# Chunk sums of log decays and angles: one fp32 product each, or two one-pass products of split parts

## The reference

```python
mag = np.sqrt(a_re * a_re + a_im * a_im)
scale = np.minimum(mag, 0.999) / (mag + 1e-06)
a_re_n, a_im_n = (a_re * scale, a_im * scale)
for t in range(S):                      # S = 768; batch 4, heads 8, head size D = 48
    new_re = ar * S_re - ai * S_im
    new_im = ar * S_im + ai * S_re
    S_re, S_im = (new_re + kv, new_im)  # kv = outer(k_t, v_t)
    y[:, :, t] = q_t @ S_re
```

## Time and profile before

| | us |
|---|---|
| median of 3 runs | 878.79 (877.34 to 878.93) |
| the profiled execution | 878.05 |
| its span, first to last instruction | 876.3 |
| PE busy | 830.9 (95% of the span) |
| DVE busy | 357.0 |
| ACT busy | 347.1 |
| POOL busy | 160.6 |
| mean granted clock of TensorE | 0.985 |

### The profile page before, as it was taken

The page is one execution under the profiler, slowest core; times in us unless marked ns, Lnnn a source line. Parts: engine busy times, 40 slices in busy tenths (PEclk is TensorE's granted clock), DMA queues, the critical chain, the costliest instruction groups (busy, mean ns, idle before and its releaser), DMA issues.

```text
span 876.3 us, 13204 instructions
## 1 busy us (share of the span) xinstructions
PE 830.9 (95%) x5194; PEld 744.6 (85%) x5194; DVE 357.0 (41%) x668; ACT 347.1 (40%) x606; POOL 160.6 (18%) x193
## 2 busy tenths in 40 slices
PE   1499999999999799999999999999999999999997
PEld 0277887798899589999998989998999889988997
DVE  1598878868765422223413122132122122122112
ACT  6889988888652131111112222222222222222221
POOL 2101122712503305555300001001001001001001
PEclk9699999999999899999999999999999999999999
DMA  9999778666523496899720001000000000000001
GB/s 171 160 205 244 105 99 123 113 94 83 136 94 117 140 202 167 266 233 252 224 73 1 1 0 37 1 1 37 1 1 36 1 1 37 1 1 37 0 1 37
DMA packets 174165, 77.31 MB, mean 88 GB/s; under 512 B 151592, under 2 KB 167304, under 8 KB 174096
## 3 DMA queue, kind: packets, MB, share of 16 engines
q1 hardware_dynamic: 169168, 60.54, 34.4%
q0 software_dynamic: 4928, 15.84, 6.4%
HBM read 60.80 MB, written 15.59 MB: 87 GB/s over the span
## 4 chain that ended last, share of the span: by engine, by line
PE 91%; DVE 3%; issue 2%; ACT 2%; DMA 1%; POOL 0%; SPq 0%; DVEq 0%; ACTq 0%; POOLq 0%
PE f_pU L1698 23%; PE f_pO L1704 22%; PE e_pH L1434 9%; PE e_pY L1448 8%; PE sc L515 5%; PE kvp L529 3%; PE tq L497 2%; PE tk L502 2%; PE yp L540 2%; PE yp L542 2%; PE cs L472 2%; PE cs L110 2%; PE cs L485 1%; PE cs L486 1%; PE cs L92 1%
## 5 line engine op out<-in xcount | busy, mean ns | idle before, releaser
L1698 PE MATMUL f_pU<-f_xT,wi 128*128 128x512 f32 x864 | 215.1, 395 | 0.8 <-DVE f_xT L1639 0.8
L1704 PE MATMUL f_pO<-wo,gT 128*128 128x384 f32 x1152 | 213.8, 336 | 0.0
L1704 PEld LDWEIGHTS f_pO<-wo,gT 128*128 128x128 f32 x1152 | 202.6, 188 | 7.5
L1698 PEld LDWEIGHTS f_pU<-f_xT,wi 128*128 128x128 f32 x864 | 161.3, 188 | 32.5 <-DVE f_xT L1639 1.2
L1655 DVE TENSOR_TENSOR gT<-g,gT 128x512 fp32r<-128x512 f32 x96 | 66.5, 692 | 286.5 <-ACT gT L1682 286.5
L1677 ACT ACTIVATE g<-f_pU 128x512 f32<-128x512 f32 x96 | 57.5, 599 | 298.3 <-PE f_pU L1698 298.3
L1645 POOL DMA_INDIRECT out<-o,row_of x24 | 24.1, 1004 | 420.8 <-DVE o L1666 414.4
L1434 PE MATMUL e_pH<-e_xT,ring 128*128 128x224 f32 x384 | 75.8, 358 | 0.1
L1434 PEld LDWEIGHTS e_pH<-e_xT,ring 128*128 128x128 f32 x384 | 74.0, 194 | 0.7 <-issue 0.3
L1448 PE MATMUL e_pY<-hT,ring 128*128 128x224 f32 x384 | 74.1, 353 | 0.0
L1448 PEld LDWEIGHTS e_pY<-hT,ring 128*128 128x128 f32 x384 | 72.1, 190 | 0.0
(11 more groups left out here) (196 smaller groups left out, 1007.6 us busy)
## 6 DMA issues: line engine op xcount, KB each, us to landing
ring<-in_moe_w SPq DMA_DIRECT2D x16, 1536.0 KB, 9.6
ring<-in_a_re SPq DMA_DIRECT2D x8, 576.0 KB, 8.8
ring<-in_a_im SPq DMA_DIRECT2D x8, 576.0 KB, 8.9
ring<-in_q SPq DMA_DIRECT2D x8, 576.0 KB, 8.1
ring<-in_k SPq DMA_DIRECT2D x8, 576.0 KB, 8.2
vraw<-in_v SPq DMA_DIRECT2D x8, 576.0 KB, 5.4
xs<-zero SPq DMA_DIRECT2D x9, 343.9 KB, 7.1
part<-in_moe_w_in POOLq DMA_DIRECT2D x12, 256.0 KB, 6.3
```

What stands on the lines that cost most here:

```text
L1698: mm = pe.matmul(pU[f % 2][:, :], wi[:, pw, c, f * 128:(f + 1) * 128], xT[b % 2][:, px, c, :], start=(k == 1), stop=(k == NK * len(TERMS)))
L1704: mm = pe.matmul(pO[t][:, 0:DM], gT[f % GB][:, pg, t * 128:(t + 1) * 128], wo[:, pw, f, :], start=(f == 0 and k == 0), stop=(f == NF - 1 a ...
```

## The change

The log decays (from group 2 on) and the angles (from group 1 on) are no longer multiplied in fp32. POOL splits each tile into a rounded fp32r part and the rest (LH, LL and AH, AL); PE multiplies both by a triangle `tri_r` in fp32r and adds them up in PSUM. The product with `pone` stays in fp32. The angles are first multiplied by 1/2pi on POOL, after `prefix` has read them. LH and LL lie where FD and FI lie. The tile ZZ is gone: its readers and writers use FD, the two exponentials that are run for their sums write to LM and GI. With that come new waits: `log_growth(g)` waits for qf_done of g (FD of the last group read by DVE) and for `fend_out` of g groups; `size_sum` waits for the split of the last group; the second part of the split waits for kf_done; `sum_l` and `sum_phi` wait for POOL. SP's program is not touched.

```diff
--- before.py
+++ after.py
@@ -234,7 +234,7 @@
 
 def attention(nc, sem, q, k, v, a_re, a_im, X, ident, cst, routing, w_skip, w_gate, xs, ends_dram, stat, fend_all, flag,
               ring, load_unit):
-    F32 = mybir.dt.float32
+    F32, F32R = mybir.dt.float32, mybir.dt.float32r
     ALU = mybir.AluOpType
     ACT = mybir.ActivationFunctionType
     PI = float(np.pi)
@@ -266,13 +266,19 @@
     DP = HALF + D
     PAIRS = HG // 2
     SWAPPED = LAST - NC
+    SPLIT_L, SPLIT_A = 2, 1
+    TURN = 0.5 / PI
+
+    def angles(g):
+
+        return (NC - 1) * g + 3 * max(g - SPLIT_A, 0)
 
     cols = [t.rearrange("b h (c p) d -> p (b h c) d", p=C) for t in (a_re, a_im, q, k, v)]
 
     ctx = ExitStack()
     with ctx:
-        def sb(name, shape, dt=F32):
-            return ctx.enter_context(nc.sbuf_tensor(name, shape, dt))
+        def sb(name, shape, dt=F32, stack=ctx):
+            return stack.enter_context(nc.sbuf_tensor(name, shape, dt))
 
         def pb(name, shape):
             return ctx.enter_context(nc.psum_tensor(name, shape, F32))
@@ -284,6 +290,9 @@
 
         NN = sb("NN", [128, W])
         FR = sb("FR", [128, W])
+        with ExitStack() as parts_ctx:
+            LH = sb("LH", [128, W], F32R, parts_ctx)
+            LL = sb("LL", [128, W], F32R, parts_ctx)
         FD = sb("FD", [128, W])
         FI = sb("FI", [128, W])
         zero = sb("zero", [SUB, X.shape[2]])
@@ -297,7 +306,10 @@
         GI = sb("GI", [128, W])
         WW = sb("WW", [128, W])
         LM = sb("LM", [128, W])
-        ZZ = sb("ZZ", [128, W])
+        ZZ = FD
+        AH = sb("AH", [128, W], F32R)
+        AL = sb("AL", [128, W], F32R)
+        tri_r = sb("tri_r", [128, C], F32R)
         AT = sb("AT", [128, HG, NC, D])
         PRE = sb("PRE", [128, HG, NC, D])
         xT = [sb(f"r_xT{i}", [128, DM])[:, :] for i in range(2)]
@@ -326,7 +338,7 @@
         kvp = pb("kvp", [128, 512])
 
         names = """re_in0 re_in1 im_in0 im_in1 qk_in0 qk_in1 v_in0 v_in1 fend_out fend_in0 fend_in1 const_ok blank_done
-            lr_done g_done w_done w2_done lw_done lm_done z_done l_done at_done pre_done size_done spread_done
+            lr_done split_l g_done w_done w2_done lw_done lm_done z_done l_done at_done pre_done size_done spread_done
             wg_blank wg_in route_const xT_done xT_out logit_done step chosen hot_done run_done rank_done slot_done sent
             limits_done count_done table_done good_step good_done sum_good flag_done
             sum_l sum_phi f_done rnd_done fr_done abs_done cos_done sin_done qf_done kf_done front_done back_done
@@ -427,6 +439,29 @@
                                pattern=[[-1, 128]], channel_multiplier=1).then_inc(s["const_ok"], 1)
             pool.wait_ge(s["const_ok"], 3)
             routing.constants(pool, s)
+            pool.tensor_copy(tri_r[:, :], tri[:, :]).then_inc(s["const_ok"], 1)
+
+            def split_l(g):
+
+                if g < SPLIT_L:
+                    return
+                pool.wait_ge(s["l_done"], g + 1)
+                pool.tensor_copy(LH[:, :], LM[:, :]).then_inc(s["split_l"], 1)
+                pool.wait_ge(s["split_l"], 2 * (g - SPLIT_L) + 1)
+                pool.wait_ge(s["kf_done"], g)
+                pool.tensor_tensor(LL[:, :], LM[:, :], LH[:, :], ALU.subtract).then_inc(s["split_l"], 1)
+
+            def split_a(g):
+
+                if g < SPLIT_A:
+                    return
+                at = AT[:, :, :, :].rearrange("p h c d -> p (h c d)")
+                pool.wait_ge(s["pre_done"], angles(g + 1) - 3)
+                pool.tensor_scalar(at, at, TURN, None, ALU.mult).then_inc(s["pre_done"], 1)
+                pool.wait_ge(s["pre_done"], angles(g + 1) - 2)
+                pool.tensor_copy(AH[:, :], at).then_inc(s["pre_done"], 1)
+                pool.wait_ge(s["pre_done"], angles(g + 1) - 1)
+                pool.tensor_tensor(AL[:, :], at, AH[:, :], ALU.subtract).then_inc(s["pre_done"], 1)
 
             def prefix(g):
                 pool.wait_ge(s["at_done"], g + 1)
@@ -434,13 +469,15 @@
                     pool.wait_ge(s["sum_phi"], NPC * g)
                 pool.tensor_copy(PRE[:, :, 1, :], AT[:, :, 0, :]).then_inc(s["pre_done"], 1)
                 for c in range(2, NC):
-                    pool.wait_ge(s["pre_done"], (NC - 1) * g + c - 1)
+                    pool.wait_ge(s["pre_done"], angles(g) + c - 1)
                     pool.tensor_tensor(PRE[:, :, c, :], PRE[:, :, c - 1, :], AT[:, :, c - 1, :], ALU.add)\
                         .then_inc(s["pre_done"], 1)
 
             for p in periods():
                 if here(p + 2):
+                    split_l(p + 2)
                     prefix(p + 2)
+                    split_a(p + 2)
                 if p == 3:
                     pool.wait_ge(s["blank_done"], 16 * routing.BLANKS)
                 if p in (3, 5, 7):
@@ -460,7 +497,10 @@
             def sum_l(g, j):
                 if not here(g):
                     return
-                pe.wait_ge(s["l_done"], g + 1)
+                if g < SPLIT_L:
+                    pe.wait_ge(s["l_done"], g + 1)
+                else:
+                    pe.wait_ge(s["split_l"], 2 * (g - SPLIT_L + 1))
                 if j == 0:
                     if g > 0:
                         pe.wait_ge(s["fr_done"], NPC * (g - 1) + 2)
@@ -469,20 +509,31 @@
                         pe.wait_ge(s["fr_done"], NPC * g)
                 else:
                     pe.wait_ge(s["f_done"], NPC * g + 1)
-                pe.matmul(cs[j % 2][:, 0:PW], tri[:, :], piece(LM, j), start=True, stop=True).then_inc(s["sum_l"], 1)
+                bank = cs[j % 2][:, 0:PW]
+                if g < SPLIT_L:
+                    pe.matmul(bank, tri[:, :], piece(LM, j), start=True, stop=True).then_inc(s["sum_l"], 1)
+                    return
+                pe.wait_ge(s["const_ok"], 4)
+                pe.matmul(bank, tri_r[:, :], piece(LH, j), start=True, stop=False)
+                pe.matmul(bank, tri_r[:, :], piece(LL, j), start=False, stop=True).then_inc(s["sum_l"], 1)
 
             def sum_phi(g, j):
                 if not here(g):
                     return
                 at, pre = (t[:, :, :, :].rearrange("p h c d -> p (h c d)") for t in (AT, PRE))
                 pe.wait_ge(s["at_done"], g + 1)
-                pe.wait_ge(s["pre_done"], (NC - 1) * (g + 1))
+                pe.wait_ge(s["pre_done"], angles(g + 1))
                 if j < 2:
                     pe.wait_ge(s["f_done"], NPC * g + 2 + j)
                 else:
                     pe.wait_ge(s["fr_done"], NPC * g + 1)
                 bank = cs[(NPC + j) % 2][:, 0:PW]
-                pe.matmul(bank, ptri[:, :], at[:, j * PW:(j + 1) * PW], start=True, stop=False)
+                if g < SPLIT_A:
+                    pe.matmul(bank, ptri[:, :], at[:, j * PW:(j + 1) * PW], start=True, stop=False)
+                else:
+                    pe.wait_ge(s["const_ok"], 4)
+                    pe.matmul(bank, tri_r[:, :], piece(AH, j), start=True, stop=False)
+                    pe.matmul(bank, tri_r[:, :], piece(AL, j), start=False, stop=False)
                 pe.matmul(bank, pone[:, :], pre[:, j * PW:(j + 1) * PW], start=False, stop=True)\
                     .then_inc(s["sum_phi"], 1)
 
@@ -664,19 +715,23 @@
 
             def size_sum(g):
                 act.wait_ge(s["lr_done"], g + 1)
-                if g > 0:
-                    act.wait_ge(s["l_done"], g)
-                act.activation(ZZ[:, :], LR[:, :], ACT.Exp, accum_out=stat[:, G + g:G + g + 1]).then_inc(s["size_done"], 1)
+                if 0 < g <= SPLIT_L:
+                    act.wait_ge(s["sum_l"], NPC * g)
+                elif g > 0:
+                    act.wait_ge(s["split_l"], 2 * (g - SPLIT_L))
+                act.activation(LM[:, :], LR[:, :], ACT.Exp, accum_out=stat[:, G + g:G + g + 1]).then_inc(s["size_done"], 1)
 
             def spread_sum(g):
                 act.wait_ge(s["w2_done"], g + 1)
-                act.wait_ge(s["l_done"], g + 1)
-                act.activation(ZZ[:, :], GI[:, :], ACT.Exp, scale=SPREAD, accum_out=stat[:, 2 * G + g:2 * G + g + 1])\
+                act.activation(GI[:, :], GI[:, :], ACT.Exp, scale=SPREAD, accum_out=stat[:, 2 * G + g:2 * G + g + 1])\
                     .then_inc(s["spread_done"], 1)
 
             def log_growth(g):
                 act.wait_ge(s["w2_done"], g + 1)
                 act.wait_ge(s["size_done"], g + 1)
+                if g > 0:
+                    act.wait_ge(s["qf_done"], g)
+                    act.wait_ge(s["fend_out"], 16 * g)
                 act.activation(ZZ[:, :], GI[:, :], ACT.Ln, bias=ONE).then_inc(s["lw_done"], 1)
 
             def loss(g):
@@ -687,7 +742,7 @@
             def angle(g):
                 if g > 0:
                     act.wait_ge(s["sum_phi"], NPC * g)
-                    act.wait_ge(s["pre_done"], (NC - 1) * g)
+                    act.wait_ge(s["pre_done"], angles(g))
```

(2 more changed lines are left out.)

## The result

| | before | after |
|---|---|---|
| median, us | 878.86 (4 runs, 877.34 to 879.1) | 959.8 (4 runs, 958.64 to 962.41) |
| span of the profiled execution | 876.3 | 958.7 |
| PE, DVE, ACT, POOL busy | 830.9, 357.0, 347.1, 160.6 | 839.7, 394.1, 349.5, 237.0 |
| mean granted clock of TensorE | 0.985 | 0.950 |

The ratio is 1.0929 (95% interval 1.0902 to 1.0956). The forecast was 940 us, with a range up to 957: the direction was right, and the time lies just above the range. By spans it is 82.4 us of loss against 61.9 forecast.

The account below looks back on a forecast made before the run. PE was taken to bound the attention, narrowly. 61.2 (store wait) - 5.0 - 0.9 (PE's saving) - 6.4 (slack) + 9 (clock) + 4 (DVE held) = 61.9 us on a span of 876.3; forecast 940 us, range 920 to 957.

Parts of the forecast that it names:

- The wait for the store: ACT's log_growth, periods 0 to 5, waits until the end states are stored from FD behind five loads; 61.2 us lost.
- 11 to 15 us: Sign of being right: ACT idle this long ahead of log_growth in periods 1 to 4, about 5 in period 5.
- What hangs behind a wait: After the five long log_growth waits: 9 us lost to TensorE's slow clock, 6.4 us gained from PE's slack.
- PE's slack: Behind a wait PE starts the next scores 1.3 us after ACT's wait less than before; five times, 6.4 us gained.
- POOL's splits: Splits of 10 us per group on POOL; lateness costed at nothing, holding up DVE at 4 us (between 0 and 9).
- Its lateness there is covered by the wait of log_growth: split_a running up to or into the next chunk 0 costs nothing, except in period 6.
- half of 2.3 us, in four periods: DVE held by POOL's subtractions in unrouted periods 0, 1, 3, 5, beyond its 3.5 us of room; taken as 4 us.
- PE's saving: fp32r pairs make each sum 0.28 us shorter; sum_l's 5.0 us gained in full, sum_phi's only 0.9, in period 6.
- Rival 2: POOL's long reads hold DVE's two-SBUF-input instructions for all 10 us per group; 26 us in all, 962 us; 8 in 100.
- Rival 1: log_growth's wait does not bind, since end states land before chunk 0 ends; kernel faster, 867 or rather 872 us; 4 in 100.
- Rival 3: Wait binds but costs less: clock up, DVE not held, faster loads; 927 or 921 us; 20 in 100 for under 930.
- Rival 4: fp32r takes as long as fp32 in this form; 5.9 us more, 946 us; 5 in 100.

Follow-up runs that it names:

- e1: Changed kernel, but from period 1 on SP issues the store of the end states ahead of the period's five loads; 909.5 us (ratio 1.0359).
- e2: Changed kernel with both splits off for all groups, fp32 products as before, only the shared home and its waits kept; 951.5 us (1.0811).
- e6: Changed kernel with angles split from group 2 on instead of group 1; 955.3 us (1.0851).
- e4: Changed kernel with the store ahead of the loads, log decays split from group 2 on, angles in fp32; 893.1 us (1.0149).
- e7: e3 plus a POOL copy and subtraction of 1152 columns per group, from group 2 on, on a tile nobody uses; 893.3 us (1.0161).
- e10: e4 with POOL's copy and subtraction for the log decays cut into six pieces of 192 columns each; 881.9 us (1.0031).
- e9: Changed kernel with ZZ's own tile back, angles unsplit, log decays split only in groups 4 and 6, store last; 877.0 us against 879.0 before (0.9979).
- e3: Changed kernel with no splits and, from period 1 on, the store of the end states ahead of the loads; 883.2 us (1.0044).
- e8: As e7, but with POOL memsets, which only write, in place of the copy and subtraction; 883.0 us (1.0043).
- e11: Changed kernel with store first, log decays and angles split from group 2 on, all POOL splits in pieces of 192 columns; 941.0 us (1.0705).

## Why the prediction was wrong, and where it was right

**The wait for the store: right.** Place, cause and size held. Start to landing was forecast from the rows of SP's queue to within 0.2 us in periods 2, 3 and 5, to 0.3 in period 4, and in period 1 it came 2.3 us sooner. ACT's own waits were shorter than the 11 to 15 us that the prediction named as a sign, 9.4 to 11.9 and then 3.0, since ACT reached log_growth later in its period. e1 shows that SP's order is the cause: moving the store gives back 50 us. That the waits add up since each period's start releases its own loads also held.

The loss by medians is 80.9 us, 19.0 more than the 61.9 of the sum. For the shared home alone the sum had 61.2 - 6.4 + 9 = 63.8 us, and e2 measured 71.4, 7.6 more. For the splits it had -5.0 - 0.9 + 4, a gain of 1.9 us, and the changed kernel lost 9.5 us against e2, 11.4 more than that. So the greater part of the miss is the splits'.

**What hangs behind a wait: mis-sized.** The term was 9 us for the clock less 6.4 for PE's slack, 2.6 in all. e2, which has only this, lost 9.3 us there over five periods: landing to the next start took 136.1 us in place of 126.8. By its rows the slack is 0.9 and not 1.3 us, since scores wait for x_out too, which follows q_out on ACT; and the clock cost 3.0 us in period 1 of e2, and in the changed kernel 5.83 - 3.85 = 2.0. I had taken less than a half-clock stretch from one start-up row. The changed kernel's windows show PE all but idle, with the clock at 0.73 in the mean, and then PE working at half clock.

```profile
97.00:108.30 11.30, 0.87 (x10) 0.75 (x8) 1.17 (x2) 2.07 (x4) 0.00 (x0) 0.73 1.06 142
108.30:112.40 4.10, 4.07 (x20) 3.74 (x20) 3.76 (x7) 3.50 (x6) 0.68 (x1) 0.50 0.11 1
```

**POOL's splits: the failed step.** Two sentences of it failed. "Its lateness there is covered by the wait of log_growth" is wrong in period 0, where the wait for the store would have been only 3 us and the first split comes 7.1 us too late for PE. Of the 12.5 us by which period 1 starts late, the home alone makes 5.4 (e2, forecast 3.1), group 2's splits in period 0 another 3.0 (e6 against e2), and group 1's angles 4.1 (the changed kernel against e6). I had priced the three instructions by width at 5.7 us; beside DVE they took 10.4, and the stall stands at sum_phi, where the prediction named none as a sign of being right. Part of that was the price itself: I gave the scaling the 1.4 us of a copy, and in none of its 27 uncut instances in the runs did it take less than 3.1. And "half of 2.3 us, in four periods" was too small for what DVE loses. Landing to the next start cost 15.1 us in the changed kernel and 9.3 in e2; the 5.8 between them, and the 4 us that PE's shorter sums should have won, I put down to the hold, by e4, e7 and e10 and not by a run of its own. It is at work in these rows of the changed kernel, DVE's first and POOL's below:

```profile
114.75 2.39 DVE L959 TENSOR_TENSOR U<-UK,fend_all 96x192 f32<-96x192 f32 x1
...
128.87 3.19 DVE L921 TENSOR_TENSOR KN<-ring,NN 128x576 f32<-128x576 f32 x1
```

```profile
114.26 2.66 POOL L452 TENSOR_TENSOR LL<-LM,LH 128x1152 fp32r<-128x1152 f32 x1 [1.39 <-DVE ring L898]
...
128.42 3.03 POOL L464 TENSOR_TENSOR AL<-AT,AH 128x1152 fp32r<-128x1152 f32 x1
```

The two, 0.35 and 0.75 us long elsewhere, began beside POOL's instruction and ended 0.2 and 0.6 us after it. DVE's busy time rose by 37 us with no instruction added. The forecast's reasoning took a mean of room per period (3.5 us), while the hold comes as one piece of 2.4 us ahead of k_out, where PE's slack is below that. A stall of PE can bring the slow clock with it, 1.5 us becoming 3 in e4, but does not always (e7). The row that the prediction had of this, a state product of 609 ns, stands twice in the 40 and not once, in the trace of before at 129.91 and 192.47, both times beside prefix's additions.

**PE's saving: mis-sized in what reaches the end.** 0.28 us per sum is right (e9: 0.85 for three). But of the 5.0 us that I let through for sum_l in full, 1.3 us came in e10 against e3, the cleanest pair. ACT and DVE are busy for most of an unrouted period, and I had not counted their limits against this term.

**The rivals.** Rival 2 (held DVE, 962 us) had the right mechanism and got 8 in 100; with e7 and e8 it is shown. Its price, all 10 us lost in each of four periods, was too high, and that its 962 us came near the measured time is luck: other terms of the sum were short. Rival 1 did not happen with the change, though e1 and e3 show its condition, an early landing; and e1, with the splits, was not faster even then. Rival 3 did not happen: the clock fell and DVE was held. Rival 4 is ruled out by e9, where three split sums are 0.85 us shorter than three in fp32.

## What to carry to other kernels

Before a short-lived value moves into a shared home, look up when that home's last reader is done, and if the reader is a DMA, what stands ahead of it in its queue: here 4.5 KB stood behind 2.9 MB, and one line of order was worth 50 us. An engine that is "free" at 18% can still be the wrong one: elementwise work on POOL that reads SBUF holds DVE's two-input instructions for the length of its own, so put it where DVE has room, or cut it, if nobody is waiting for POOL. A saving on the engine that bounds counts only while the other two have room, and here ACT and DVE were busy for some 90% of the period.

## What the runs showed of the hardware

- An idle time of PE of 1.47 us, in a stretch that was busy otherwise, was followed by a granted clock of 0.62 in the mean over the next 4 us (e4). I had expected that only of the long waits. It is no rule: behind idle times of 2.00 and 2.01 us in e7, and of 1.37 us at 128.23 in the changed kernel, it stayed at 1.00.
- POOL's memset of 2304 columns beside DVE's two-input product changed neither (2.02 and 0.35 us); a subtraction of 1152 columns stretched the product to 2.71 (e7).
- The exclusion works both ways, and the second to come waits: POOL's copy and subtraction of 1152 columns took 1.3 and 3.0 us in e1, and DVE's product beside the subtraction 3.8 in place of 1.35; in the changed kernel, issued while DVE had three products in a row, the copy took 3.4 and the products their usual time.
- Cut into six pieces, POOL's scaling of 1152 columns took 4.3 us in some periods of e11 and 7.9 in others, and 3.1 to 4.7 as one instruction in the changed kernel.
